# Second softmax of a fused attention and gating kernel: one chain of operations per unit in place of one for both units

## What is computed

```python
def sm_attn(qq, kk, vv):
    s = scale * np.matmul(qq, kk.transpose(0, 1, 3, 2))
    s = s - np.max(s, axis=-1, keepdims=True)
    a = np.exp(s)
    a = a / (np.sum(a, axis=-1, keepdims=True) + 1e-09)
    return np.matmul(a, vv)
p_packed = sm_attn(p, k, v)          # first softmax, over 576 keys
x = sm_attn(q, p_packed, p_packed)   # second softmax, over 32 packed rows
gate = 1 / (1 + np.exp(-gate_pre(x)))   # 5-tap causal convolution of x
y = (gate * (x @ w_val)) @ w_out
h = np.maximum(y @ w_in, 0); u, v = h[..., :512], h[..., 512:]
v_n = (v - mean(v)) / np.sqrt(var(v) + 1e-06)
out = (u * (w_spatial @ v_n + b_spatial)) @ w_out2
```

## Time and profile before

| | |
|---|---|
| median of 3 runs | 624.9 us (624.13 to 625.7) |
| the profiled execution | 626.42 us, span 624.6 us from first to last instruction |
| PE busy | 569.7 us, 91% of the span |
| DVE busy | 457.6 us, 73% |
| ACT busy | 308.9 us, 49% |
| mean granted TensorE clock | 0.967 of full speed |

### The profile page before, as it was taken

One profiled execution on the slowest core, in us unless ns is written; L12 is line 12 of the kernel. 1 busy time (PEld: TensorE's weight loads), 2 busy tenths in 40 slices (PEclk: granted clock), 3 DMA queues, 4 the chain that ended last, 5 costly groups with the idle time before them and its releaser, 6 DMA issues.

```text
span 624.6 us, 11859 instructions
## 1 busy us (share of the span) xinstructions
PE 569.7 (91%) x4734; PEld 389.6 (62%) x4734; DVE 457.6 (73%) x855; ACT 308.9 (49%) x481; POOL 10.3 (2%) x16
## 2 busy tenths in 40 slices
PE   4878996999979997999969997999979999899997
PEld 3335464775757665675757665676747756576785
DVE  2569999993889648894788748894688838895541
ACT  3247656565348444555447535465445544373412
POOL 0000000000000000000000000000000000000000
PEclk9979997999989999999999999899979999799999
DMA  8930621013400322004300223004210000002001
GB/s 278 320 134 2 233 87 67 2 39 119 152 0 3 123 98 85 0 19 136 145 6 0 83 93 131 0 0 155 85 66 0 38 38 0 0 0 77 1 1 76
DMA packets 24037, 45.13 MB, mean 72 GB/s; under 512 B 1937, under 2 KB 11153, under 8 KB 22994
## 3 DMA queue, kind: packets, MB, share of 16 engines
q1 hardware_dynamic: 19410, 35.42, 17.2%
q10 hardware_dynamic: 4608, 9.44, 4.1%
HBM read 35.42 MB, written 9.44 MB: 72 GB/s over the span
## 4 chain that ended last, share of the span: by engine, by line
issue 83%; PE 13%; DVE 2%; ACT 1%; POOL 0%; POOLq 0%
PE X L453 5%; PE X L469 3%; PE X L431 2%; PE X L414 2%; PE Y L395 1%; DVE vn_l L610 0%; DVE vn L762 0%; PE Y L381 0%; POOL rstd L275 0%; ACT u_res L997 0%; PE X L419 0%; DVE u_max L774 0%; DVE prob L669 0%; DVE prob L666 0%; DVE sum L674 0%
## 5 line engine op out<-in xcount | busy, mean ns | idle before, releaser
L702 DVE SCALAR_TENSOR_TENSOR gate<-xT,conv_sb,gate 128x576 f32<-128x576 f32 x128 | 95.2, 812 | 10.2 <-ACT gate L997 10.2
L741 DVE BATCH_NORM_STATS2 bn<-vn 128x6 f32<-128x512 f32 (+1 forms) x40 | 27.6, 691 | 71.4 <-ACT vn L1060 60.3
L453 PE MATMUL X<-wsp_h,vn_h 128*128 128x288 f16 x320 | 70.8, 306 | 0.0
L453 PE MATMUL X<-wsp_l,vn_h 128*128 128x288 f16 x256 | 57.6, 310 | 0.0
L453 PE MATMUL X<-wsp_h,vn_l 128*128 128x288 f16 x256 | 57.1, 308 | 0.0
L469 PE MATMUL X<-gatedT_h,wfin_h 128*128 128x288 f16 x256 | 52.3, 286 | 0.3 <-DVE gatedT_l L611 0.3
L431 PE MATMUL X<-gvT_h,wfused_h 128*128 128x288 f16 x256 | 52.5, 287 | 0.0
L431 PE MATMUL X<-gvT_h,wfused_l 128*128 128x288 f16 x256 | 52.3, 286 | 0.0
L469 PE MATMUL X<-gatedT_h,wfin_l 128*128 128x288 f16 x256 | 52.3, 286 | 0.0
L469 PE MATMUL X<-gatedT_l,wfin_h 128*128 128x288 f16 x256 | 52.3, 286 | 0.0
L431 PE MATMUL X<-gvT_l,wfused_h 128*128 128x288 f16 x256 | 52.3, 286 | 0.0
(11 more groups left out here) (159 smaller groups left out, 1127.4 us busy)
## 6 DMA issues: line engine op xcount, KB each, us to landing
k_sb<-kT SPq DMA_DIRECT2D x16, 576.0 KB, 5.0
q_sb<-qT SPq DMA_DIRECT2D x8, 1152.0 KB, 5.2
outT<-u_res ACTq DMA_DIRECT2D x32, 288.0 KB, 2.1
v_sb<-v_rows SPq DMA_DIRECT2D x8, 1024.0 KB, 5.4
stage_b<-w_in SPq DMA_DIRECT2D x2, 1024.0 KB, 14.6
stage_b<-w_spT SPq DMA_DIRECT2D x1, 1152.0 KB
v_sb<-v_rows SPq DMA_DIRECT2D x8, 128.0 KB, 5.3
stage_a<-w_outT SPq DMA_DIRECT2D x1, 1024.0 KB, 10.5
```

The costliest lines, as they stand in the source:

```text
L453: last = mm(X[1 - c % 2][:, a, 0:HALF], x, w[:, a * HALF:(a + 1) * HALF], start=i == 0, stop=i == len(terms) - 1)
L702: tap = nc.vector.scalar_tensor_tensor(gate[:, j, :], xT[:, j, k:k + S], conv_sb[:, j, k:k + 1], gate[:, j, :], ALU.mult, ALU.add)
L741: nc.vector.bn_stats(bn6[0:rows, t, :], vn[0:rows, t, :]).then_inc(stats_ready, 1)
```

## The change

Each of the two units gets its own chain on 576 columns, unit 1 first (`UNIT_ORDER` is (1, 0)), where one chain worked on 1152 columns. ACT gets two exponentials of 576 columns. The back transposition belongs to each unit's chain. `pack_magnitudes` stands between the two units' scale parts, and `pack_gains` behind both. Since Y[0] is now turned last, PE's `packed_value` waits until both units are turned. In the first pass `late_low_spatial` stays behind the two subtractions, and the scale part of unit 1 now stands between it and `pack_magnitudes`.

```diff
             def packed_value(n, first=False):
-                pe.wait_ge(s2_turned, UNITS * n + 1)
+                pe.wait_ge(s2_turned, UNITS * n + UNITS)
...
-            def softmax2_sub(n, base):
-                dve.wait_ge(s2_done, n + 1)
-                for u in range(UNITS):
-                    nc.vector.transpose(two(prob2[:, u, :]), halves(Y[u])).then_inc(s2_turned, 1)
-                dve.wait_ge(s2_turned, UNITS * n + UNITS)
-                chain(nc.vector.tensor_reduce(max2[:, :], blocks(prob2), AX.X, ALU.max), base)
-                nc.vector.tensor_tensor(blocks(prob2), blocks(prob2), over_blocks(max2),
+            def softmax2_sub(n, i, base):
+                u = UNIT_ORDER[i]
+                if i == 0:
+                    dve.wait_ge(s2_done, n + 1)
+                nc.vector.transpose(two(prob2[:, u, :]), halves(Y[u])).then_inc(s2_turned, 1)
+                dve.wait_ge(s2_turned, UNITS * n + i + 1)
+                chain(nc.vector.tensor_reduce(stat(max2, u), blocks(u), AX.X, ALU.max), base)
+                nc.vector.tensor_tensor(blocks(u), blocks(u), over_blocks(max2, u),
                                         ALU.subtract).then_inc(sub2_ready, 1)
...
+            def softmax2_scale(n, i, base):
+                u = UNIT_ORDER[i]
+                dve.wait_ge(exp2_ready, UNITS * n + i + 1)
+                chain(nc.vector.tensor_reduce(stat(sum2, u), blocks(u), AX.X, ALU.add), base)
+                chain(nc.vector.tensor_scalar(stat(sum2, u), stat(sum2, u), SUM_EPS, 1.0 / PROB_GAIN,
                                               ALU.add, ALU.mult), base)
-                chain(nc.vector.reciprocal(rsum2[:, :], sum2[:, :]), base)
-                nc.vector.tensor_tensor(blocks(prob2), blocks(prob2), over_blocks(rsum2),
+                chain(nc.vector.reciprocal(stat(rsum2, u), stat(sum2, u)), base)
+                nc.vector.tensor_tensor(blocks(u), blocks(u), over_blocks(rsum2, u),
                                         ALU.mult).then_inc(prob2_ready, 1)
-
-            def prob2_turn(n):
-                dve.wait_ge(prob2_ready, n + 1)
-                for u in UNIT_ORDER:
-                    nc.vector.transpose(prob2T_f[:, u, :], prob2[:, u, :]).then_inc(prob2_turned, 1)
+                dve.wait_ge(prob2_ready, UNITS * n + i + 1)
+                nc.vector.transpose(prob2T_f[:, u, :], prob2[:, u, :]).then_inc(prob2_turned, 1)
...
-                softmax2_sub(n, base)
+                softmax2_sub(n, 0, base)
+                softmax2_sub(n, 1, base)
                 if first:
                     late_low_spatial()
-                    pack_magnitudes(n)
-                    softmax2_sums(n, base)
-                else:
-                    softmax2_sums(n, base)
-                    pack_magnitudes(n)
+                softmax2_scale(n, 0, base)
+                pack_magnitudes(n)
+                softmax2_scale(n, 1, base)
                 pack_gains(n, base)
-                softmax2_scale(n, base)
-                prob2_turn(n)
...
-                softmax2_exp(n)
+                softmax2_exp(n, 0)
+                softmax2_exp(n, 1)
```

More of the change, by code:

```diff
@@ L654, in pack_low @@
                 low(pval_l[:, :, :], packed_val[:, :, :], pval_h[:, :, :], gain_pack[:, 1:2]).then_inc(pack_split, 1)
[L657 to L661, removed]
-            def softmax2_sub(n, base):
-                dve.wait_ge(s2_done, n + 1)
-                for u in range(UNITS):
-                    nc.vector.transpose(two(prob2[:, u, :]), halves(Y[u])).then_inc(s2_turned, 1)
-                dve.wait_ge(s2_turned, UNITS * n + UNITS)
-                chain(nc.vector.tensor_reduce(max2[:, :], blocks(prob2), AX.X, ALU.max), base)
-                nc.vector.tensor_tensor(blocks(prob2), blocks(prob2), over_blocks(max2),
-                                        ALU.subtract).then_inc(sub2_ready, 1)
@@ L672, in softmax2_sums, with blocks, stat @@
[L672 to L677, removed]
+            def blocks(u):
+                return prob2[:, u, :].rearrange("p (s c) -> p s c", c=NP)
+            def stat(tile, u):
+                return tile[:, u * BLOCKS:(u + 1) * BLOCKS]
@@ new lines, in over_blocks @@
+            def over_blocks(tile, u):
+                return stat(tile, u).unsqueeze(2).to_broadcast([P, BLOCKS, NP])
+            def softmax2_sub(n, i, base):
[6 more added lines that the diff above has]
+                nc.vector.tensor_tensor(blocks(u), blocks(u), over_blocks(max2, u),
+                                        ALU.subtract).then_inc(sub2_ready, 1)
@@ L873, in _ @@
             pack_pairs(0)
[L874 to L877, removed]
+            softmax2_sub(0, 0, 0)
+            softmax2_sub(0, 1, 0)
+            softmax2_scale(0, 0, 0)
+            softmax2_scale(0, 1, 0)
             pack_magnitudes(0)
@@ L1016, in read_packed_value, with softmax2_exp @@
                 copy(packed_val[:, u, :], Y[0][:, u, 0:D]).then_inc(pv_ready, 1)
-            def softmax2_exp(n):
-                act.wait_ge(sub2_ready, n + 1)
-                nc.scalar.activation(prob2[:, :, :], prob2[:, :, :], ACT.Exp, scale=SCALE).then_inc(exp2_ready, 1)
+            def softmax2_exp(n, i):
+                u = UNIT_ORDER[i]
+                act.wait_ge(sub2_ready, UNITS * n + i + 1)
+                nc.scalar.activation(prob2[:, u, :], prob2[:, u, :], ACT.Exp, scale=SCALE).then_inc(exp2_ready, 1)
             def high_packed(n):
@@ L1129, in _ @@
             read_packedT(0)
-            softmax2_exp(0)
+            softmax2_exp(0, 0)
+            softmax2_exp(0, 1)
             read_fused(0, 1)
@@ L1236, in steps_per_batch @@
 def steps_per_batch(chunks, taps, units):
-    max1, pack, softmax2, variance = 1 * units, 2 * units, 1 + 3, 2
+    max1, pack, softmax2, variance = 1 * units, 2 * units, (1 + 3) * units, 2
     pack_gains, gated_gains, undo = 3, 1 + 3, 1
```

## The result

| | before | after |
|---|---|---|
| median of 20 runs each | 625.31 us (623.99 to 626.87) | 627.25 us (624.87 to 629.6) |
| ratio after / before | | 1.0033, 95% interval 1.0023 to 1.0042 |
| profiled execution (its span) | 626.42 us (624.6) | 627.32 us (625.5) |

The kernel has become 0.33% slower, some 2 us. The forecast was 1.2 us faster (623.7, range 621.8 to 627.0); the measured time is on the other side and 0.25 us above the range.

The account below looks back on a forecast made before the run. DVE's chain was taken to bound each pass up to `attention_out`, PE the rest. Prologue −0.2, first pass +2.4, three passes −0.8, passes 5 to 7 −2.6 gave −1.2 us: 623.7 us, range 621.8 to 627.0.

Parts of the forecast that it names:

- What bounds the kernel: Each pass: DVE's chain sets the part the change touches; PE sets the rest, from `attention_out` to the next pass.
- The cost of the halves: DVE's wide operations: 0.75 us for each of 576 columns against 1.35 for 1152, so halving saves 0.61 us.
- cheap halves: Rival, DVE: 576 columns take 0.68 us, six passes gain 0.6 us each, 620.1 us; chance 0.03.
- The loop pass: Passes 2 to 7: `attention_out` at T+18.17, 0.28 us earlier each; T is the start of DVE's first transposition.
- The late exponential: Rival, ACT: unit 1's exponential isn't done at T+4.51, a 0.3 us hole returns six times, 625.5 us; chance 0.07.
- The first pass: First pass: row sums 3.14 us later, `attention_out` 2.4 us later, bounds 1.2 and 3.0.
- The prologue: Ahead of the first pass: the exponential's hole goes, two parts come, L636 starts 0.18 us earlier; 0.2 us saved.
- The clock: Passes 5 to 7: PE's idle pieces, 2.4 and 1.6 us, are too short for a fall; each wins 0.6 us.
- the three signs: Signs against it: PE late at `attention_out`; L639 waiting for `packed_val`; first pass costing under 1.2 or over 3 us.
- The slow rival: Rival, loop: slow clock stays and PE is late at `attention_out`; 627.6 us, or 631.4 with all six slow; chance 0.18.
- the three stops: PE's waits in a loop pass: before `packed_value`, before the row sums, before `attention_out`; one may bring the slow clock.

Follow-up runs that it names:

- the three kernels with these waits: The changed kernel (1.0033), the changed kernel with the first pass's `pack_magnitudes` early (1.008), and the changed kernel with one chain in the first pass (1.0027).
- both units turned first: The changed kernel with both units transposed before either's reductions, so `packed_value` waits for Y[0] alone again: 627.67 us, 1.0044 of before.
- the kernel before with its first wait filled: The kernel before with 13 pairs of useless matmuls at the start of `u_chunk(b, 3)` in loop passes: 628.35 us, 1.0046 of before.
- the kernels with the early read: DVE's read of the `u_max` sums put ahead of `gated(b, 0)`: changed kernel 0.9938, with one chain in the first pass 0.9886, kernel before 0.9975.
- the kernel with early magnitudes: The changed kernel with `pack_magnitudes` back directly behind `late_low_spatial` in the first pass: 630.33 us, 1.008 of before.

## Why the prediction was wrong, point by point

**What bounds the kernel: right.** DVE's chain from T to L780, and PE from there on.

**The cost of the halves: right.** The four wide operations of a unit (L672, L673, L679, L683) take 0.74 to 0.76 us each, as taken from the earlier trace rows; two of them, and the reciprocal:

```profile
L673 DVE TENSOR_TENSOR prob<-prob,max 128x576 f32<-128x576 f32 x16 | 12.1, 758 | 0.6
...
L679 DVE TENSOR_REDUCE sum<-prob 128x18 f32<-128x576 f32 x16 | 11.9, 742 | 0.0
L682 DVE RECIPROCAL rsum<-sum 128x18 f32<-128x18 f32 x16 | 4.3, 266 | 0.5
```

The rival "cheap halves" is refuted by these. An instruction that waits for the one ahead starts 0.79 us behind it (L672 at 311.71, L673 at 312.50), one that doesn't wait 0.68 us (L673 at 314.77, L679 at 315.45). The fixed cost of 75 ns that the Trainium skill's page "Vector Engine (DVE) Microarchitecture Reference" gives under "Rate slope and fixed cost" would have had 0.68. It is given there after queue overlap, and the trace agrees with it only from start to start and only where nothing is waited for.

**The loop pass: right to 0.03 us.** Row sums at T+8.88 (foretold 8.88), gains at T+11.53 (11.53), `packed_value` at T+3.19 (3.16), `attention_out` at T+18.14 (18.17). The late exponential didn't happen. That passes 5 to 7 would win the slow clock's 0.6 us on top held in the trace as well: 0.81 to 0.94.

**The first pass: right in size.** 2.65 us, foretold 2.4 with 1.2 to 3.0 as its bounds, and PE is late at `attention_out` there as foretold. The idle time ahead of the row sums did not stay above 4.85 us, it was 4.06; a slow stretch followed all the same.

**The prologue: right for what the change does** (from T to the row sums 0.14 less in the trace, 11.64 and 11.78, foretold 0.2).

**The clock: wrong, and the sum fell with it.** The step that failed is the sentence that the new idle pieces are shorter than 2.64 us, that a wait of that length was not followed by a fall, and that the passes would therefore keep 2.4 GHz. One row of a trace was read as a rule. In the changed kernel the piece of 2.42 us is followed by a fall in four of six loop passes: the granted clock from `packed_value` to the row sums is 0.70, where the prediction wanted 1.00. That was covered and cost nothing. In the two passes without it the wait of 1.87 or 1.88 us ahead of `attention_out` is followed by a fall. The term that was missing in the sum is the number of falls behind `attention_out` by 1.62 us each: two in the profiled execution, two to four by the ratios with and without the wait. None of the three signs that the prediction named for being wrong has come; it had looked for none behind `attention_out`.

**The slow rival: the right suspect in the wrong place.** It named the three stops, but priced the fall by a stretch of before that lies ahead of the row sums, 0.44 to 1.08 us, with PE late at L780 as the point from which it decides. No loop pass of the changed kernel came late there. Its 627.6 is close to the measured 627.25 by accident. (For all six passes its terms add up to 6.8 and 631.7, not 6.5 and 631.4, and the range that I gave ends at 627.0, below the rival's own figure.) I had counted that PE is 1.9 us early at `attention_out` as cover; it was the wait that did the harm. In the kernel before the slow clock ahead of the row sums used up just this slack, and the last waits of passes 5 to 7 were 0.46 us; taking the first slow stretch away made the second possible.

**Where the slow clock should have been looked for.** Its price could be read from the trace of before: 22 matmuls in 5 us at 0.50 against 43 to 47 at full speed, and a part of the pass without one wait. A fall of 3.4 us there has to cost half of it. That is 1.7 us, and 1.62 was measured. What that trace couldn't tell is how often a wait of 1.9 us is followed by a fall. The Trainium skill's page "TensorE: Matmul & The Clock Gate", section "HAM oscillation — how this bites in real kernels", counts the penalty as half of the throttled time. For PE's own work the trace agrees: in pass 5 of before the clock was low for 6.8 us, 5.8 of them with PE at work, and that work took 2.8 us longer. What the kernel loses depends on who is the bound: there it was 0.6 us, behind `attention_out` all of the 1.62.

## What to carry to other kernels

A wait of the matmul engine has two prices, its own length and the slower clock that may follow, and the second is charged to whatever comes next. So look at what stands *behind* each wait: a stop ahead of work that another engine covers is nearly free, the same stop ahead of the stretch where PE is the bound costs half of every slow microsecond. When a change shortens PE's path up to a wait without moving what it waits for, it lengthens the wait: either shorten the releasing chain (here by moving a read of 0.15 us forward by one operation, 6 us in the end) or leave the stop where it was.

## What the runs showed that was not expected

- Useless matmuls made a kernel faster: 60 of them in six passes (5 pairs each) brought the changed kernel from 1.0033 to 0.9954 of before.
- Equal waits are followed by either clock. 3.38 us: slow in five of six loop passes of before, fast in one; 1.87 and 1.88 us: slow in pass 4, fast in pass 5. In the second case the trace shows what differs: in all 18 passes of the three kernels with these waits the fall came behind `attention_out` exactly when none had come ahead of the row sums. It is no rule for other waits: with 3.67 us ahead of the row sums (both units turned first) one pass kept full clock throughout, its 1.88 us wait included. With 2.64 us in the kernel before with its first wait filled, the clock had been full in all six passes, and it fell in three; what decides there is open.
- Behind a wait of 0.46 to 1.46 us ahead of `attention_out` (the kernels with the early read, and those with filled waits) no loop pass was slow in the profiled executions.
- Slow stretches in the passes came in two lengths, about 3.4 and 6.8 us, and cost 1.6 and, in the first pass of the kernel with early magnitudes, 2.7 us behind `attention_out`.
- The mean granted clock doesn't rank executions or kernels. In the kernel before, the faster executions mostly have the higher clock (623.56 us at 0.981, 627.12 at 0.962), but two executions of the changed kernel with 0.978 each took 624.87 and 627.93 us. That this comes from where the slow stretches lie is likely after the experiments, but those two weren't profiled.
